# Expert results in two token halves, with a new order in POOL's loop, in a fused attention and mixture-of-experts kernel

## The reference

```python
state = 0                                   # per batch (4) and head (8), 48 x 48
for t in range(768):                        # linear attention with decay w and bonus u
    y[:, :, t] = r_t @ (state + (u*k_t) v_t^T)
    state = w * state + k_t v_t^T
x = y as 3072 tokens x 384
h = x @ w_in                                # 384 -> 2048
x = (h * sigmoid(h)) @ w_out                # 2048 -> 384
logits = x @ w_gate + modality_bias[modality_id]      # 8 experts
e = argmax(logits);  gate = softmax(logits)[e]
out = gate * (relu(x @ w1[e]) @ w2[e])      # 384 -> 1024 -> 384, each token by its own expert
```

## Time and profile before

| | |
|---|---|
| runs, median (lowest to highest) | 816.91 us (814.11 to 817.08) |
| the profiled execution: its time, its span | 810.66 us, 809.1 us |
| PE busy | 755.2 us, 93% |
| DVE, ACT, POOL busy | 515.4, 432.0, 225.9 us |
| experts block | about 555 us to the end |
| PE's last matmul ends | 794.93 us |

### The profile page before, as it was taken

The page is one execution under the profiler, slowest core; times in us unless marked ns, Lnnn a source line. Parts: engine busy times, 40 slices in busy tenths (PEclk is TensorE's granted clock), DMA queues, the critical chain, the costliest instruction groups (busy, mean ns, idle before and its releaser), DMA issues. The chain is left out here.

```text
span 809.1 us, 24921 instructions
## 1 busy us (share of the span) xinstructions
PE 755.2 (93%) x9890; PEld 736.4 (91%) x9890; DVE 515.4 (64%) x1367; ACT 432.0 (53%) x1075; POOL 225.9 (28%) x337
## 2 busy tenths in 40 slices
PE   2599999999999999999999999997999999999993
PEld 2599899999999999999998999997899999999992
DVE  7758865685558666766576657424866666566561
ACT  3456463745565545555564546434655655566561
POOL 4421222152214122422224211202324322223321
PEclk9999999999999999999999999997999999999997
DMA  8921222222221222222222210132596766655661
GB/s 319 409 89 38 73 94 73 94 74 93 75 91 43 90 73 93 74 94 73 93 75 61 94 59 12 50 148 71 173 224 212 242 243 210 251 206 197 231 203 70
DMA packets 24159, 104.90 MB, mean 130 GB/s; under 512 B 4411, under 2 KB 9800, under 8 KB 20482
## 3 DMA queue, kind: packets, MB, share of 16 engines
q1 hardware_dynamic: 19362, 93.30, 33.4%
q0 software_dynamic: 4704, 10.29, 4.3%
HBM read 93.86 MB, written 10.11 MB: 129 GB/s over the span
## 5 line engine op out<-in xcount | busy, mean ns | idle before, releaser
L575 ACT ACTIVATE g<-ps_h 128x256 f32<-128x256 f32 x192 | 73.4, 383 | 195.3 <-PE ps_h L893 146.4
L891 PE MATMUL ps_h<-x_hi,wi_hi 128*128 128x256 f32 x576 | 164.6, 286 | 0.0
L892 PE MATMUL ps_h<-x_lo,wi_hi 128*128 128x256 f32 x576 | 162.2, 282 | 0.0
L893 PE MATMUL ps_h<-x_hi,wi_lo 128*128 128x256 f32 x576 | 162.0, 281 | 0.0
L908 PE MATMUL ps_o<-wo_hi,g_hi 128*128 128x392 f32 x384 | 135.4, 353 | 3.6 <-DVE g_lo L746 3.0
L909 PE MATMUL ps_o<-wo_lo,g_hi 128*128 128x392 f32 x384 | 130.5, 340 | 0.0
L910 PE MATMUL ps_o<-wo_hi,g_lo 128*128 128x392 f32 x384 | 130.5, 340 | 0.0
L746 DVE TENSOR_TENSOR g_lo<-g,g_hi 128x256 fp32r<-128x256 f32 x192 | 83.3, 438 | 66.9 <-ACT g_hi L568 65.0
L473 POOL TENSOR_TENSOR store<-store,up_half 128x256 f32<-128x256 f32 x44 | 34.2, 778 | 286.1 <-PE ps_y L878 282.0
L891 PEld LDWEIGHTS ps_h<-x_hi,wi_hi 128*128 128x128 f32 x576 | 109.8, 191 | 1.8 <-issue 1.1
L893 PEld LDWEIGHTS ps_h<-x_hi,wi_lo 128*128 128x128 f32 x576 | 110.1, 191 | 0.0
(11 more groups left out here) (193 smaller groups left out, 1563.3 us busy)
## 6 DMA issues: line engine op xcount, KB each, us to landing
store<-in_w SPq DMA_DIRECT2D x28, 1536.0 KB, 7.1
store<-in_quads SPq DMA_DIRECT2D x48, 704.0 KB, 4.7
x_rows<-rows SPq DMA_DIRECT2D x12, 384.0 KB, 3.2
wi_raw<-in_wi SPq DMA_DIRECT2D x4, 768.0 KB, 10.5
woT_raw<-in_woT SPq DMA_DIRECT2D x4, 768.0 KB, 11.9
wo_raw<-in_wo SPq DMA_DIRECT2D x4, 768.0 KB, 12.5
store<-x_rows,entries POOLq DMA_INDIRECT x26
out_rows<-y,entries_out POOLq DMA_INDIRECT x26, 6.8
```

Source lines behind the costliest of these rows:

```text
L575: S.activation(g[:, F % 2, :], ps_h[F % 2][:, 0:ETOK], ACT.Silu).then_inc(g_made, 1)
L891: T.matmul(out, hi, x_hi[:, t % 2, c, :], start=(c == 0), stop=False)
L892: T.matmul(out, hi, x_lo[:, t % 2, c, :], start=False, stop=False)
L893: last = T.matmul(out, lo, x_hi[:, t % 2, c, :], start=False, stop=(c == KC - 1))
```

## The change

In the words of its author: expert results go out by token half; PE's down step takes one half of 128 tokens at a time, POOL's loop does entries first and its last scatters follow the loop. PE finishes half 0 over all chunks, signals `half_summed`, turns the next rows, and does half 1. ACT scales each half by itself (`y_half`, `y_made`). POOL waits before each scatter for its half. SP waits in each iteration for `y_out` of the tile before and counts that in `results_landed`, which POOL's last copy of entries waits for; SP also takes over the last wait for the results.

```diff
 SP
+            sp.sem_inc(results_landed, 1)
             tile(z.first_tiles, 0)
             with sp.Fori(1, z.ETILES) as j:
                 with sp.If(j < tiles):
                     tile(table, j)
+                    sp.wait_ge(y_out, 16 * EB * j)
+                    sp.sem_inc(results_landed, 1)
             sp.wait_ge(w1_in, 16 * tiles)
             sp.wait_ge(w2_in, 16 * tiles)
+            sp.sem_inc(sp_passed, 1)
+            sp.wait_ge(y_out, 16 * EB * tiles)
             sp.sem_inc(sp_passed, 1)
 POOL
+            def last_entries():
+                pool.wait_ge(results_landed, tiles)
+                pool.sem_inc(pool_passed, 1)
+                nc.gpsimd.tensor_copy(entries_out[:], entries_next[:]).then_inc(entries_kept, 1)
+
             def results_out(j):
-                pool.wait_ge(y_made, j + 2)
-                pool.sem_inc(pool_passed, 1)
                 for i in range(EB):
+                    pool.wait_ge(y_half if i == 0 else y_made, j + 1 if i == 0 else j + 2)
+                    pool.sem_inc(pool_passed, 1)
                     nc.gpsimd.indirect_dma_start(...)
-            tile(table, 1, False)
             with pool.Fori(2, z.ETILES) as j:
                 with pool.If(j < tiles):
+                    tile(table, j - 1, False)
                     pool.wait_ge(entries_in, 16 * (j + 1))
                     gather(j)
                     results_out(j - 1)
-                    tile(table, j, False)
+            pool.wait_ge(x_gathered, 16 * EB * tiles)
+            pool.sem_inc(pool_passed, 1)
+            last_entries()
             results_out(tiles - 1)
-            pool.wait_ge(entries_in, 16 * (tiles + 1))
-            pool.wait_ge(y_out, 16 * EB * tiles)
-            pool.sem_inc(pool_passed, 1)
 ACT
+                act.wait_ge(half_summed, j + 1)
+                act.wait_ge(entries_kept, j + 1)
+                nc.scalar.activation(y[:, 0, :], ps_y[0][:, 0:DM], ACT.Copy, scale=...).then_inc(y_half, 1)
                 act.wait_ge(y_summed, j + 2)
-                act.wait_ge(entries_kept, j + 1)
-                for i in range(EB):
-                    last = nc.scalar.activation(y[:, i, :], ps_y[i][:, 0:DM], ACT.Copy, scale=...)
-                last.then_inc(y_made, 1)
+                nc.scalar.activation(y[:, 1, :], ps_y[1][:, 0:DM], ACT.Copy, scale=...).then_inc(y_made, 1)
 PE
-                for f in range(FCH):
-                    if f == (FCH - 2 if first else FCH // 2):
+                for i in range(EB):
+                    for f in range(FCH):
+                        if i == 1 and f == (FCH // 2 if first else 0):
                             ...
                             pe.wait_ge(x_gathered, 16 * EB * (j + 1))
                             turn()
-                    pe.wait_ge(h_lo_made, FCH * j + f + 1 + 4)
-                    ...
-                    for i in range(EB):
+                        if i == 0:
+                            pe.wait_ge(h_lo_made, FCH * j + f + 1 + 4)
+                            ...
                         T.matmul(...)  # three, as before
-                last.then_inc(y_summed, 1)
+                    last.then_inc(half_summed if i == 0 else y_summed, 1)
```

More of the change, by code:

```diff
@@ L1032, in experts_block @@
         y_made = sem("y_made")
+        y_half = sem("y_half")
+        results_landed = sem("results_landed")
+        half_summed = sem("half_summed")
         y_out = sem("y_out")
@@ L1235, in tile @@
                 x_high(j + 1)
+                act.wait_ge(half_summed, j + 1)
+                act.wait_ge(entries_kept, j + 1)
+                nc.scalar.activation(y[:, 0, :], ps_y[0][:, 0:DM], ACT.Copy, scale=entries_out[:, 0, 1:2].bitcast(F32)).then_inc(y_half, 1)
                 act.wait_ge(y_summed, j + 2)
-                act.wait_ge(entries_kept, j + 1)
-                for i in range(EB):
-                    last = nc.scalar.activation(y[:, i, :], ps_y[i][:, 0:DM], ACT.Copy, scale=entries_out[:, i, 1:2].bitcast(F32))
-                last.then_inc(y_made, 1)
+                nc.scalar.activation(y[:, 1, :], ps_y[1][:, 0:DM], ACT.Copy, scale=entries_out[:, 1, 1:2].bitcast(F32)).then_inc(y_made, 1)
             x_high(0)
@@ L1283, in tile @@
                 pe.wait_ge(y_made, j + 1)
-                for f in range(FCH):
-                    if f == (FCH - 2 if first else FCH // 2):
[L1286 to L1289, removed]
-                    pe.wait_ge(h_lo_made, FCH * j + f + 1 + 4)
-                    if f % (FCH // PIECES) == 0:
-                        pe.wait_ge(w2_lo_made, PIECES * j + f // (FCH // PIECES) + 1)
-                    for i in range(EB):
+                for i in range(EB):
+                    for f in range(FCH):
+                        if i == 1 and f == (FCH // 2 if first else 0):
+                            if first:
+                                pe.wait_ge(ranks_read, 1)
+                            pe.wait_ge(x_gathered, 16 * EB * (j + 1))
+                            turn()
+                        if i == 0:
+                            pe.wait_ge(h_lo_made, FCH * j + f + 1 + 4)
+                            if f % (FCH // PIECES) == 0:
+                                pe.wait_ge(w2_lo_made, PIECES * j + f // (FCH // PIECES) + 1)
                         hi, lo = (x[:, f, i * P:(i + 1) * P] for x in (h_hi, h_lo))
```

## The result

The changed kernel takes 822.33 us (median of 10 runs, 818.5 to 826.17), the kernel before, run beside it, 815.17 us (10 runs). The ratio is 1.007, with a 95% interval of 1.0047 to 1.0093: slower by 0.7%, 5.7 us by the ratio and 7.2 by the medians. The time lies in the range of the prediction (810.5 to 824), but not where it was thought likeliest: the forecast case reached from 813.5 to 821, "no measurable change" had 0.48, "slower" 0.29. All medians and ratios in this document leave out two executions far from the rest, one of experiment 1 (4122.19 us) and one of the kernel before beside experiments 6 and 7 (1878.84 us).

The account below looks back on a forecast made before the run. PE was taken to bound the experts block; stalls of +6.15 us less 5.5 us of shorter ending gave +0.6 us, added to the 816.91 us median for 817.5 us, with an 8-in-10 range of 810.5 to 824.

Parts of the forecast that it names:

- the forecast case: Whole kernel: mean stall of 0.4 to 1.1 us per tile, ending 4.5 to 6.5 us shorter; chance 0.48.
- no measurable change: Whole kernel: time not told apart from before, a difference of about 0.5% or 4.1 us being measurable; chance 0.48.
- slower: Whole kernel: measurably slower than the kernel before; chance 0.29.
- The mechanism: Experts tiles: SP's wait delays w1 by 1.4 to 1.9 us, entries and gathers follow, rows fall behind w2, PE stalls.
- The lead of 0.8 us: Experts tiles: the second gather must be issued at least some 0.8 us before the w2 load to avoid a stall.
- POOL's reordered loop: Experts block: same sequence, cut elsewhere; no half goes out earlier in the steady state, two long-met waits cost some 0.1 us each.
- The ending: From PE's last matmul to the span's end: 8.65 us against 14.17, so 5.5 gained (4.5 to 6.5).
- The 7.15: Start of last scatter to span's end: 8.2 us before, with half of a possible 2.1 saving assumed.
- The stall: PE waiting for gathered rows: 0.75 us in each of ten tiles, less tile 10's existing 1.35, making +6.15.
- rival 2: Experts tiles: larger stalls, mean from 1.15 us, slow w2 loads adding 1.9; 823.6 us, or 827; chance 0.24.
- The third: Kernel's end: the ending does not shrink, with stalls as forecast; +6, 823 us; chance 0.05.
- The first: Experts tiles: no stalls, PE waits for nothing; -6.9, 810.0 us; chance 0.23.

Follow-up runs that it names:

- experiment 1: The kernel before with only SP's wait for the previous tile's results added ahead of the next w1 load; 826.71 us, ratio 1.0135.
- experiments 6 and 7: 6 has its own line; 7: kernel before, both halves together, with the changed kernel's POOL loop and ending, results wait on DVE; ratio 0.9948, repeated 0.9946.
- experiment 6: The changed kernel with POOL, too, waiting for the last results to land before leaving the block; executed once, 820.05 us.
- experiment 3: The changed kernel, SP's wait kept, with SP also waiting before each w1 load until the tile's entries have landed; 807.93 us, ratio 0.9912.
- experiment 5: The changed kernel with the results wait on DVE instead of SP and each w2 load about one us later by a fixed delay; 803.75 us, ratio 0.9911.
- experiment 4: The changed kernel with the results wait on DVE instead of SP, each w2 load waiting for the next tile's gathered rows; ratio 0.9881, repeated 0.9936.

## Why the prediction came out as it did

**The mechanism was right.** SP's wait holds the w1 load (predicted U+15.55 to 16.0, measured U+15.6 to 16.4, and U+17.5 and 17.6 where the results came late); the entries follow w1; the second gather meets the w2 load (predicted after U+5.3 and near U+6.2, measured U+6.22 in eight of the ten tiles); the w2 load comes earlier (predicted U+6.11, measured U+6.26); the stall settles in nine of ten tiles; only the longest one, tile 8's, gave the next tile enough time. Experiment 1 shows the cause by itself, 3 that the order of entries and w1 carries it, 5 that the order of the second gather and the w2 load decides. Two figures in this chain were less sure than they look. The lead of 0.8 us was read from two tiles, and experiment 1 has stalls with a lead of up to 0.96. And the second gather was expected near U+6.2 because the stall would move it there; in eight tiles it was held at U+6.22 wherever between U+4.26 and U+4.78 the first gather began (last section), so that the two figures agree is in part luck. POOL's reordered loop did nothing in the steady state, as argued, and PE's new order cost nothing: a tile without a stall takes 17.39 in both.

**The ending was right**: 8.42 against 8.65 predicted; the last scatter 1.5 behind PE, and 6.9 from there against 7.15. The 7.15 was luck in part, half of a saving of 2.1 or none. POOL's own last step is the end of its last issue, 0.97 behind its start, and not the start, so leaving early saves 1.3 (experiment 6).

**The stall was sized too small**, and this is the step that put the likeliest time at +0.6 us instead of the measured 5.7 by the ratio. It said: "If both gathers are behind the load they travel together and the cast comes some 0.3 sooner relative to it, by my estimate, a stall of 0.6. I take 0.75." The stalls of tiles 3 to 12, by the start of ACT's cast less U+13.42, are 1.57, 1.23, 0.94, 0.92, 1.24, 2.31, 0, 0.89, 2.35 and 2.38 us, 1.38 in the mean. The case of both gathers behind the load never came: the first was always ahead of it (U+3.52 to 5.59). Three things make up the difference.

- In the six tiles with a quick load the cast came 8.05 to 8.71 after the w2 load, never sooner than 8.05; one row, tile 10's 8.18, was taken as typical and then even bettered.
- In tiles 8, 11 and 12 it came 9.46 to 9.53 after it, behind slow w2 loads (9.2, 9.0 and 8.8 us to landing, 6.4 to 8.0 in the others). The worst of the w2 loads shown took 9.1 instead of 7.2, but the forecast case left them out and only rival 2 had them. Before, a slow w2 load did not delay the rows of its own tile, which had gone ahead of it. It could cost the next tile something: the one stall, in tile 10, follows the slow load of tile 9 (9.1 us), behind which the results were copied only at U+16.33, so that the entries and gathers of tile 10 came late. Now the delay lands on PE in the same tile.
- Tile 8 lost another 1.59 us to the clock (last section).

Ten times 0.75, less 1.35, was 6.15; it became 14.16. By the medians less came of it, since the profiled execution of the kernel before is a quick one, 4.5 us below its median.

**Rivals.** The second rival, stalls of 1.15 and more in the mean, is what happened, and its 823.6 is nearest to the 822.33 measured. One of its reasons held, slow w2 loads, in three tiles and not two; the other did not, for the w2 load did come earlier. The third, an ending that does not shrink, is excluded. So the stated range held because it reached to the second rival's value, not because the forecast case came true. The first, no stalls, is excluded for the changed kernel, but by experiment 5 it is nearly what the change gives without SP's wait and with the lead restored: the 6.9 us predicted for it compare with 6.2 by the medians (809.93 to 803.75).

## What to carry to other kernels

A wait put on a queue that "has time" must be priced by what stands behind it in that queue and by what shares the DMA engines with it: here the 1536 KB load could be late for free, but a 2 KB load behind it could not, and the rows behind that were the ones PE needed. Where small transfers that somebody waits for share the engines with large ones, look at the lead of each over the next large load, tile by tile; and count the lead to the end of the small one's issue, not to its start. If the large load has slack, let it wait. A fixed delay of about one us and a wait for the rows themselves both served here, and their times are not told apart; a large load that goes much later can hold up what follows it, here the results and with them ACT.

## What the runs showed of the hardware

**A gather's issue stretches beside DVE's pieces.** The first gather of tile 6 took 1.66 us to issue instead of about 1, and the second started at 683.08, just when DVE's last piece of w2 ended (682.15+0.95 = 683.10), which also released the w2 load (683.12). In eight tiles of the changed kernel the second gather stands at U+6.22, whenever between U+4.26 and U+4.78 the first had begun. Before, it stood at U+5.34 (659.67) in most tiles, and there, too, a piece of DVE's ended at that moment (658.74+0.95 = 659.69):

```profile
658.74 0.95 DVE L1167 TENSOR_TENSOR w_lo<-store,w_hi 128x768 fp32r<-128x768 f32 x1
```

So the lead is not lost gradually: a first gather that is late by half a us makes the second miss one piece of DVE's and go in a dead heat with w2. The Trainium skill (SBUF — State Buffer, SBUF: two separate sides) says that a DVE operation with two SBUF inputs and a GpSimd operation that reads SBUF exclude each other at a shared port pair for a whole instruction; its warning there, on descriptors that GpSimd cannot write meanwhile, speaks of another kind of DVE operation. The rows agree with this in part. Before, the second gather of tile 5 (659.67 to 660.62) ran beside most of a piece (659.94 to 660.89) and took the usual 0.95. No run here moved DVE's pieces away from the gathers to show it.

**A small load behind a large one comes in with it.** In the changed kernel the entries load was issued 0.84 us after the w1 load (674.97 and 674.13) and landed 5.3 after its own issue; with nothing in front (experiment 3) it landed after 2.2. The Trainium skill (DMA: Bandwidth & Descriptors, Queues, rings and completion order) has engines change between queues only after a whole packet. The trace shows a turn at least as coarse; how many descriptors or packets a load has, no view here shows.

**A stall can cost the clock.** Behind the 2.31 us stall of tile 8, windows of the changed kernel:

```profile
729.20:731.00 1.80, 1.80 (x10) 1.80 (x9) 0.56 (x1) 1.40 (x3) 0.37 (x2) 0.71 0.02 7
731.00:733.00 2.00, 2.00 (x7) 2.00 (x7) 0.47 (x2) 0.04 (x1) 0.73 (x1) 0.50 0.52 98
```

The granted clock is 0.50 (1.2 of 2.4 GHz) from 731 to 733, and the tile loses 1.59 us beyond its stall (21.29-17.39-2.31). The clock fell in the same way behind stalls of 3.1 and 3.5 us in experiment 1 (tiles 3 and 11), of 2.5 and 3.8 in experiment 6 (tiles 5 and 11), and of 2.6 in the repeat of experiment 4 (tile 3, where PE waited for h and not for rows), and 0.8 to 1.6 us more were lost each time. It did not fall behind the 2.35 and 2.38 of tiles 11 and 12 here, nor behind the 3.3 of tile 12 in experiment 5. So the length of the stall alone does not decide it; what does was not tried. This cost is part of the difference between kernels that stall and kernels that do not, and the forecast had no term for it.
